# A fused convolution and rational feed-forward kernel: chunk groups of 3,3,2,3,3,2 instead of 3,2,3,3,2,3, and the transposes beside groups 2 and 5

## What is computed

```python
h = x @ w_in                                    # 192 -> 2048
P = a[0] + a[1]*h + a[2]*h*h + a[3]*h*h*h
Q = 1.0 + abs(b[0])*abs(h) + abs(b[1])*h*h
out = (P / (Q + 1e-6)) @ w_out                  # 2048 -> 192
```

## Time and profile before

| | |
|---|---|
| runs | 1422.62, 1422.70, 1420.06 us |
| profiled execution | 1420.86 us, its span 1419.1 us |
| granted TensorE clock, mean | 0.992 |
| PE busy | 1307.0 us, 92% |
| ACT busy | 1270.7 us, 90% |
| DVE busy | 1214.8 us, 86% |
| POOL busy | 1036.6 us, 73% |

### The profile page before, as it was taken

How to read it: one execution, slowest core, us unless ns; L and a number is a source line. 1 busy time by engine, 2 the same in 40 slices (tenths; PEclk the granted TensorE clock), 3 DMA queues, 4 the chain that set the end, 5 groups by cost and what they waited for, 6 DMA issues and landing times.

```text
span 1419.1 us, 19150 instructions
## 1 busy us (share of the span) xinstructions
PE 1307.0 (92%) x6912; PEld 1178.2 (83%) x6912; DVE 1214.8 (86%) x872; ACT 1270.7 (90%) x1030; POOL 1036.6 (73%) x672
## 2 busy tenths in 40 slices
PE   0279999999999999999999999999999999999997
PEld 0268898888898888889888888988888888888897
DVE  2988898899889889989888998988988898898775
ACT  1278999999999999999999999999999999999995
POOL 1878787787878778878777887877788787787210
PEclk9889999999999999999999999999999999999999
DMA  2534444534544544454454354445345445533432
GB/s 89 144 90 110 103 117 114 128 85 107 131 94 114 125 117 88 115 120 105 109 131 107 87 126 108 117 109 131 87 102 131 97 117 120 119 83 81 100 68 67
DMA packets 35486, 152.21 MB, mean 107 GB/s; under 512 B 3992, under 2 KB 10260, under 8 KB 35472
## 3 DMA queue, kind: packets, MB, share of 16 engines
q0 software_dynamic: 18432, 100.67, 34.9%
q1 hardware_dynamic: 16752, 51.36, 10.5%
q10 hardware_dynamic: 288, 0.00, 0.0%
HBM read 38.78 MB, written 12.58 MB: 36 GB/s over the span
## 4 chain that ended last, share of the span: by engine, by line
PE 62%; ACT 25%; issue 7%; DVE 4%; DMA 2%; SPq 0%; ACTq 0%; DVEq 0%
PE ops L690 33%; PE hps L680 28%; ACT num L479 7%; ACT beta L474 6%; ACT den L452 6%; ACT den L471 4%; DMA xwin<-in_x 2%; ACT out_sb L446 2%; PE hps L665 1%; DVE gate L543 1%; DVE conv L554 1%; ACT den L455 1%; DVE gate L605 0%; DVE wi_lo L561 0%; DVE num L621 0%
## 5 line engine op out<-in xcount | busy, mean ns | idle before, releaser
L690 PE MATMUL ops<-wo,gate 128*128 128x192 f32 x4096 | 702.2, 327 | 41.7 <-ACT out_sb L446 35.8
L690 PEld LDWEIGHTS ops<-wo,gate 128*128 128x128 f32 x4096 | 676.0, 191 | 69.8 <-issue 48.5
L621 DVE TENSOR_TENSOR num<-num,hps 128x1536 f32<-128x1536 f32 (+1 forms) x192 | 301.6, 1571 | 153.4 <-ACT num L479 153.4
L327 POOL TENSOR_TENSOR conv<-conv,prod 128x768 f32<-128x768 f32 (+2 forms) x192 | 395.2, 2058 | 15.0
L605 DVE SCALAR_TENSOR_TENSOR gate<-num,coef,den 128x1536 f32<-128x1536 f32 (+1 forms) x192 | 375.0, 1953 | 2.6 <-issue 1.6
L323 POOL TENSOR_TENSOR prod<-xwin,taps 128x768 f32<-128x768 f32 (+2 forms) x192 | 336.7, 1754 | 3.4
L624 DVE SCALAR_TENSOR_TENSOR num<-num,coef,hps 128x1536 f32<-128x1536 f32 (+1 forms) x192 | 314.2, 1637 | 6.8
L346 POOL DMA_DIRECT2D den<-beta x128 | 112.7, 881 | 265.8 <-ACT beta L474 260.3
L479 ACT ACTIVATE num<-hps,coef 128x1536 f32<-128x1536 f32 (+1 forms) x192 | 287.8, 1499 | 0.0
L452 ACT ACTIVATE den<-den,one_eps 128x1536 f32<-128x1536 f32 (+1 forms) x192 | 277.8, 1447 | 0.0
L471 ACT ACTIVATE den<-hps,absb 128x1536 f32<-128x1536 f32 x128 | 196.6, 1536 | 77.1 <-PE hps L680 70.5
(11 more groups left out here) (52 smaller groups left out, 766.5 us busy)
## 6 DMA issues: line engine op xcount, KB each, us to landing
den<-beta POOLq DMA_DIRECT2D x128, 768.0 KB, 5.6
xwin<-in_x SPq DMA_DIRECT2D x30, 960.0 KB
out<-out_sb SPq DMA_DIRECT2D x32, 384.0 KB, 3.8
taps_raw<-in_weight_gen SPq DMA_DIRECT2D x32, 112.0 KB, 3.9
wo<-in_moe_w_out SPq DMA_DIRECT2D x1, 1536.0 KB, 13.6
num<-in_moe_w_in SPq DMA_DIRECT2D x2, 512.0 KB, 6.6
num<-in_moe_w_in SPq DMA_DIRECT2D x4, 256.0 KB, 7.9
xwin<-in_x SPq DMA_DIRECT2D x1, 768.0 KB
```

Of the source, the lines that this page charges most:

```text
L327: pool.tensor_tensor(conv[parity][:, cols], conv[parity][:, cols], prod[k % 2][:, cols], ALU.add).then_inc(conv_steps, 1)
L621: dve.tensor_tensor(slot(num, g), slot(num, g), h_of(q), ALU.mult).then_inc(num2_ready, 1)
L690: last = pe.matmul(ops[:, j // 2, (j % 2) * D:(j % 2 + 1) * D], gate[:, g % GATE_RING, n * COLS + j * P:n * COLS + (j + 1) * P], wo[:, c, ...
```

## The change

The groups are 3,3,2,3,3,2. The two-chunk groups are now q = 2 (banks 0 and 1, so bank 2 is free) and q = 5 (banks 3 and 4, bank 5 free). Part 1 is transposed beside group 2 into bank 2, part 0 beside group 5 into bank 5. The groups whose sum is made by DMA are 0, 1, 3 and 4. The special place of tile 0 is gone, with its waits and its special calls.

```diff
-GROUP_CHUNKS = (3, 2, 3, 3, 2, 3)
+GROUP_CHUNKS = (3, 3, 2, 3, 3, 2)
...
-DMA_GROUPS = (0, 2, 3, 5)
-BANK0, BANK1 = 2, 5
-XT0, XT1 = 4, 1
-FIRST_XT1 = 2
+DMA_GROUPS = (0, 1, 3, 4)
+BANK0, BANK1 = 5, 2
+XT0, XT1 = 5, 2
...
-                    if first and q == FIRST_XT1 - 1:
-                        hi_part1(t + 1, 1 - odd, ops[:, 0, :])
...
-                    if xt_ahead and q == (FIRST_XT1 if first else XT1):
+                    if xt_ahead and q == XT1:
...
-                    if xt_ahead and not first and q == XT1 + 2:
+                    if xt_ahead and q == XT1 + 2:
                         pe.wait_ge(xt_lo_ready, 2 * t + 3)
...
                     if first and q == LAG:
-                        pe.wait_ge(xt_lo_ready, 3)
                         pe.wait_ge(wo_loaded, 16)
```

More of the change, by code:

```diff
@@ L415, in hi_part0, with hi_part1 @@
                 act.activation(xt_hi[parity][:, :], hps[:, BANK0, :], ACT.Copy).then_inc(xt_hi_ready, 1)
-            def hi_part1(s, parity, bank):
+            def hi_part1(s, parity):
                 act.wait_ge(xt_ps1, s + 1)
-                act.activation(xt_hl[parity][0:D1, :], bank[0:D1, :], ACT.Copy).then_inc(xt_hi_ready, 1)
+                act.activation(xt_hl[parity][0:D1, :], hps[0:D1, BANK1, :], ACT.Copy).then_inc(xt_hi_ready, 1)
             for s in range(2):
@@ L434, in _ @@
                 act.activation(wi_hi[:, :, units], wi_stage[:, :, units], ACT.Copy).then_inc(wi_hi_ready, 1)
-            hi_part1(0, 0, hps[:, BANK1, :])
+            hi_part1(0, 0)
             hi_part0(0, 0)
@@ L462, in tile @@
                         hi_part0(t + 1, 1 - odd)
-                    if xt_ahead and q == XT1 and not first:
-                        hi_part1(t + 1, 1 - odd, hps[:, BANK1, :])
+                    if xt_ahead and q == XT1:
+                        hi_part1(t + 1, 1 - odd)
                     if not first or q >= RING:
@@ L568, in lo_part0, with lo_part1 @@
                                   ALU.subtract).then_inc(xt_lo_ready, 1)
-            def lo_part1(s, parity, bank):
+            def lo_part1(s, parity):
                 dve.wait_ge(xt_hi_ready, 2 * s + 1)
-                dve.tensor_tensor(xt_hl[parity][D1:P, :], bank[0:D1, :],
+                dve.tensor_tensor(xt_hl[parity][D1:P, :], hps[0:D1, BANK1, :],
                                   xt_hl[parity][0:D1, :].bitcast(F32), ALU.subtract).then_inc(xt_lo_ready, 1)
@@ L591, in _ @@
             pre_softmax_start(2, 0)
-            lo_part1(0, 0, hps[:, BANK1, :])
+            lo_part1(0, 0)
             lo_part0(0, 0)
@@ L613, in tile @@
                         lo_part0(t + 1, 1 - odd)
[L614 to L617, removed]
+                    if xt_ahead and q == XT1:
+                        lo_part1(t + 1, 1 - odd)
                     if not first or q >= GATE_LAG:
@@ L660, in transpose0, with transpose1 @@
                 last.then_inc(xt_ps0, 1)
-            def transpose1(parity, bank):
+            def transpose1(parity):
                 for j in range(TOK):
-                    last = pe.transpose(bank[0:D1, j * P:(j + 1) * P],
+                    last = pe.transpose(hps[0:D1, BANK1, j * P:(j + 1) * P],
                                         conv[parity][:, j * D + P:(j + 1) * D], ident[:, :])
@@ L712, in tile @@
                         pe.sem_inc(pe_passed, 1)
-                        transpose1(1 - odd, ops[:, 0, :] if first else hps[:, BANK1, :])
-                    if xt_ahead and not first and q == XT1 + 2:
+                        transpose1(1 - odd)
+                    if xt_ahead and q == XT1 + 2:
                         pe.wait_ge(xt_lo_ready, 2 * t + 3)
@@ L734, in _ @@
             pe.wait_ge(conv_by_dve, CONV_STEPS)
-            transpose1(0, hps[:, BANK1, :])
+            transpose1(0)
             transpose0(0)
```

## The result

The changed kernel takes 1433.61 us (median of 4 runs, 1433.34 to 1436.25) against 1422.22 us for the kernel before (4 runs). The ratio is 1.009, with a 95% interval from 1.0074 to 1.0106: slower by about 11 us. The profiled execution took 1433.44 us, its span 1431.6.

The account below looks back on a forecast made before the run. A ring through PE and ACT bounds the kernel. Loop 28 x (1.07 - 0.40) = +18.8 us, last two cycles -0.8, start -3, tail -2: +13 on 1420.86, forecast 1434 us, range 1404 to 1443.

Parts of the forecast that it names:

- What bounds the kernel: Each tile of the old kernel: a ring of 27.82 us on PE and 13.87 on ACT, period 41.69.
- The hand-over moved to group 3: PE to ACT in each tile: a period of 41.29 us, 0.40 less than before, if nothing else stalls.
- The start of the two scalings: After `back` of group 0: POOL's L353 at 9.35 us, DVE's small L639 at 9.56, waiting until POOL ends.
- `xt_lo` seen by PE at 11.64: Counted from PE's start of `back` 0: `xt_lo` made at 11.58 us and seen at 11.64, wanted at 10.81.
- 0.83 us late and 0.24 for the refill: PE's wait for `xt_lo` and its refill behind it: together 1.07 us more in every tile with a tap sum.
- The sum of the loop: Tiles 1 to 28: 28 x (1.07 - 0.40) = +18.8 us; the last two cycles, without tap sum: -0.8.
- Start and tail: Both ends of the kernel: start between 0 and -6 us, taken as -3; tail between 0 and -4, taken as -2.
- the wait for a gate and the slow group behind it: First cycle: PE's 2.21 us wait and a group of 5.81 instead of 4.14, which the new order may escape.
- The wait for the evacuation: PE's `back` of group 0 still waits for ACT's evacuation in the changed kernel, about 0.75 us.
- Costs of nothing: Loop: `xt_hl` of part 1, the regrouped sums, the gates and SP's stores and loads hold no engine.
- The first rival: DVE's small scaling gets in ahead of or beside POOL's and takes 0.18 us, PE isn't held: 1404; chance 0.21.
- The second rival: POOL's convolution step also goes before DVE's small scaling, `xt_lo` 1.6 us later: about 1479; chance 0.04.

Follow-up runs that it names:

- Run 6: The kernel before, with only ACT's evacuation moved ahead of Ln in iteration 3: 1388.27 us, 0.977 of the kernel before.
- run 1: The changed kernel with DVE's tap sum moved from the end of iteration 4 to the end of iteration 5: 1400.51 us, 0.985 of the kernel before.
- run 2: The changed kernel with `xt_lo` at the end of iteration 4 and the tap sum right behind it on DVE: 1400.39 us, ratio 0.985.
- Run 3: The changed kernel with POOL's scaling of group 5 waiting for the end of DVE's tap sum: 1410.24 us, ratio 0.992.
- run 4: The changed kernel with ACT's evacuation ahead of Ln in iteration 3: 1471.28 us, ratio 1.036.
- run 7: The changed kernel with POOL's scaling of group 5 waiting for the tap sum and ACT's evacuation ahead of Ln: 1414.99 us, ratio 0.996.
- run 5: The changed kernel with the tap sum at the end of iteration 5 and ACT's evacuation ahead of Ln: 1389.46 us, ratio 0.978.

## Why the prediction was right

- **What bounds the kernel**: PE and ACT in a ring, with 1.16 us of wait in it. Run 6 shows that the wait was the ring's and could be had: 33 us less.
- **The hand-over moved to group 3, 41.29 us a tile without a stall**: runs 1 and 2 measured 41.28.
- **The start of the two scalings, 9.35 and 9.56**: measured 9.36 and 9.58. POOL first: right in the 28 tiles that the sum prices. In tile 0, which the sum leaves out, DVE was first and met another POOL instruction. `xt_lo` seen by PE at 11.64: measured 11.65, from two small errors that cancel (it is made at 11.52 instead of 11.58, and the hand-over to PE takes 0.13 instead of 0.06).
- **0.83 us late and 0.24 for the refill, a period of 42.36**: measured 0.85, 0.26 and 42.39. The sum of the loop was +18.0, measured +19.4.
- **Start and tail**: -3 and -2 were middles of wide bounds; measured -4.3 and -2.6. The first cycle did escape the wait for a gate and the slow group behind it, as was hoped, but tile 0 has a tap sum too, and its wait for `xt_lo` stands nowhere in the sum: 2.93 us, and a product of 5.31. So the first cycle grew, and the start is shorter only by what came before it. In the tail the eight chunks were taken at their old 12.08 us; they took 10.67, since the clock didn't fall. The two terms fell on opposite sides of the loop's error, and the total, +13, met +12.6 for the profiled executions and +11.4 for the medians. That it came so near is partly luck: the parts were off by 1.4, 1.3 and 0.6.
- **The wait for the evacuation, 0.75 us**: measured 0.76 (23.7 over 31).
- **Costs of nothing**: no wait of PE for `h_used` or a gate is left in the loop in the list of waits (their 1 to 3 entries are start and end). DVE's gates stretched in new places (2.81 us at 748.78), with no one waiting.
- **The first rival's price was wrong.** It said 1404 if DVE's scaling ran free, with PE not held, by a margin of 0.06 us between 10.75 and 10.81. Run 3 is that case as far as `xt_lo` goes: 1410, since the margin came out at -0.03 and the refill was paid. The step that failed: it set the moment at which `xt_lo` is there (10.75; measured 10.70) against the one at which PE runs dry, and left the hand-over to PE out, which takes 0.13 (724.09 to 724.22 in run 3). It would still have been faster.
- **The rule of the Trainium skill** (SBUF — State Buffer, section "SBUF: two separate sides") that the port pair shared by VectorE and GpSimd is locked for whole instructions agrees with the traces of the changed kernel and of runs 2 and 3: 1.00, 0.42 and 0.18 us for the same 32 values, by how much of POOL's scaling was left. The second rival, two turns for POOL, didn't come: the waiting instruction got the port next, each time.

## What to carry to other kernels

When a producer is moved to just before its consumer, list what stands between them on the producer's engine, and give each small item the length it has when another engine holds its memory port, not its length alone. Put the urgent instruction first: here one exchange of two neighbours was worth 33 us of 1433. And before shortening a wait, follow the ring it lies on; if another wait lies on the same ring, the time goes there.

## What was not expected

- In run 4, after 1.97 us without work, PE's granted clock fell in 21 of 28 tiles (0.68 over 3.4 us in the tile at 710.63), and 15 matmuls took 5.3 us instead of 3.75; in the other seven, after the same wait, it stayed at 1.00. After 0.84 to 0.86 us (the changed kernel) and 1.16 us (run 7) it did not fall in any tile. In the changed kernel a wait of 2.93 us in tile 0 was followed by a fall (5.31 us), and one of 2.44 us ahead of the last eight chunks was not (10.67 us). The length of the wait alone doesn't say what follows. So a wait that grows from 1 to 2 us can cost more than its own length, and run 4 lost most of its time over the changed kernel that way.
- Being late by 0.03 us costs PE 0.29: the next product takes 3.75 instead of 3.49 us once PE has run dry, and it is the same 3.75 after pauses of 0.03 (run 3), 0.31 (run 5), 0.84 (the changed kernel) and 1.16 us (run 7).
